# A clustered-attention kernel: masks turned earlier, conversions moved to a head's begin, and the value scale found in other places

## What is computed

```
q_assign, k_assign = argmax over 16 centroids of the normalized dot products
mask   = q_assign[:, :, :, None] == k_assign[:, :, None, :]
scores = where(mask, q k^T / 8, -1e9)
attn   = exp(scores - max(scores)); attn /= sum(attn) + 1e-9
x      = attn v                        # 16 heads, put side by side: 1536 x 512
x      = x + gate * relu(x w1[e]) w2[e]           # 1st layer, one expert e per token, if x w_skip > 0
out    = gate * sigmoid(x w_out[e]) * relu(x w1[e]) w2[e]       # 2nd layer
```

## Time and profile before

| | |
|---|---|
| median of 3 runs | 782.02 us |
| the profiled execution | 782.19 us |
| its span in the trace | 780.5 us |
| TensorE matmul busy | 713.3 us |
| VectorE busy | 447.1 us |
| ScalarE busy | 342.0 us |
| GpSimd busy | 277.7 us |
| first exponential of head 0 | 39.26 us |
| first exponential of head 15 | 347.07 us |
| last of attention on VectorE (L506) starts | 360.31 us |

### The profile page before, as it was taken

The page is one execution under the profiler, slowest core; times in us unless marked ns, Lnnn a source line. Parts: engine busy times, 40 slices in busy tenths (PEclk is TensorE's granted clock), DMA queues, the critical chain, the costliest instruction groups (busy, mean ns, idle before and its releaser), DMA issues.

```text
span 780.5 us, 17315 instructions
## 1 busy us (share of the span) xinstructions
PE 713.3 (91%) x5937; PEld 587.2 (75%) x5946; DVE 447.1 (57%) x916; ACT 342.0 (44%) x681; POOL 277.7 (36%) x341
## 2 busy tenths in 40 slices
PE   7888898888888888888899999999899999999996
PEld 4566676666767666766489999985499999999985
DVE  5767757777676777755663665444734434444321
ACT  2377667776666666665321333113212321412300
POOL 2156666555555555554121222220111312121211
PEclk8999989999999999999999999999999999999998
DMA  7101111111111111289165699729246364673100
GB/s 226 42 3 41 42 42 40 40 40 40 40 40 40 40 40 40 77 321 359 47 238 195 250 343 344 243 106 334 82 148 232 146 247 160 247 262 127 41 30 28
DMA packets 45969, 105.49 MB, mean 135 GB/s; under 512 B 5459, under 2 KB 11603, under 8 KB 45936
## 3 DMA queue, kind: packets, MB, share of 16 engines
q1 hardware_dynamic: 36352, 87.60, 31.9%
q0 software_dynamic: 4544, 12.70, 5.0%
q10 hardware_dynamic: 5040, 4.77, 1.9%
HBM read 87.64 MB, written 13.11 MB: 129 GB/s over the span
## 4 chain that ended last, share of the span: by engine, by line
PE 47%; DVE 2%; DMA 2%; issue 1%; ACT 0%; POOL 0%; POOLq 0%; ACTq 0%; DVEq 0%
PE hT_ps_layer L1132 24%; PE y_ps_layer L1145 6%; PE y_ps_layer L1149 6%; PE y_ps_layer L1152 6%; PE x_turn_layer L1119 2%; DMA x<-x_mid 1%; PE hT_ps_layer L1074 1%; PE hT_ps_layer L1061 1%; PE hT_ps_layer L1059 1%; PE x_turn_layer L1049 1%; DVE row_one_hot_layer L961 0%; DMA x_tile_layer<-x_src,token_to_read_layer 0%; DMA x_mid<-y_out_layer,y_token_layer 0%; PE count_ps_layer L1049 0%; PE rank_ps_layer L1049 0%
## 5 line engine op out<-in xcount | busy, mean ns | idle before, releaser
L349 POOL TENSOR_TENSOR probs_lo<-probs,probs_hi 128x384 f16<-128x384 f32 x160 | 143.6, 922 | 151.6 <-ACT probs_hi L305 151.6
L1132 PEld LDWEIGHTS hT_ps_layer<-xT_layer,w 128*128 128x128 f32 x1664 | 189.6, 192 | 3.4 <-DVE xT_layer L994 1.3
L1132 PE MATMUL hT_ps_layer<-xT_layer,w 128*128 128x128 f32 x1664 | 190.2, 275 | 0.5 <-issue 0.5
L883 ACT ACTIVATE hT_hi_layer<-hT_ps_layer 128x512 fp32r<-128x512 f32 x52 | 31.0, 597 | 238.8 <-PE hT_ps_layer L1132 238.8
L465 DVE TENSOR_REDUCE max_halves<-turn 128x1 f32<-128x384 f32 x192 | 99.6, 553 | 48.0 <-PE turn L565 44.4
L304 ACT ACTIVATE probs<-scores 128x384 f32<-128x384 f32 x192 | 102.8, 535 | 33.0 <-PE scores L586 32.6
L305 ACT ACTIVATE probs_hi<-scores 128x384 f16<-128x384 f32 x192 | 104.5, 545 | 0.0
L604 PE MATMUL pv<-v_hi_and_one,probs_hi 128*128 128x65 f16 x576 | 63.0, 198 | 26.2 <-ACT probs_hi L305 25.3
L1021 DVE SCALAR_TENSOR_TENSOR hT_lo_layer<-hT_ps_layer,hT_hi_layer 128x512 fp32r<-128x512 f32 x52 | 34.6, 689 | 88.5 <-ACT hT_hi_layer L883 77.4
L565 PE MATMUL turn<-kB,qB 96*128 96x384 f32 x192 | 79.1, 422 | 3.0 <-DVE max_halves L465 1.5
L878 ACT ACTIVATE w_hi<-w 128x1024 fp32r<-128x1024 f32 x64 | 62.4, 1046 | 27.0 <-issue 27.0
(11 more groups left out here) (214 smaller groups left out, 1100.5 us busy)
## 6 DMA issues: line engine op xcount, KB each, us to landing
w<-in_moe_w_dram SPq DMA_DIRECT2D x32, 2048.0 KB, 9.3
w<-in_v_dram ACTq DMA_DIRECT2D x4, 768.0 KB, 5.7
qk_raw<-in_q_dram SPq DMA_DIRECT2D x16, 192.0 KB, 2.7
qk_raw<-in_k_dram SPq DMA_DIRECT2D x16, 192.0 KB, 2.8
qB<-qA SPq DMA_DIRECT2D x16, 192.0 KB, 2.7
kB<-kA SPq DMA_DIRECT2D x16, 192.0 KB, 3.1
x_src<-x SPq DMA_DIRECT2D x2, 1536.0 KB, 11.2
x_mid<-x SPq DMA_DIRECT2D x2, 1536.0 KB, 14.4
```

The costliest lines, as they stand in the source:

```text
L349: nc.gpsimd.tensor_tensor(p_lo[slot][:, half], probs[slot][:, half], p_hi[slot][:, half], ALU.subtract).then_inc(p_lo_pool, 1)
L1132: t = nc.tensor.matmul(hp[n][:, i * P:(i + 1) * P], W1[par][:, c, f * P:(f + 1) * P], xT[:, c, :], start=(c == 0), stop=(c == CD - 1))
```

## The change

- TensorE: in each key tile the high weighing of both halves comes first, then the scores of tile kt+2, then the low weighing of tile kt-1; before, low and high weighing alternated and the scores came last. The table `BETWEEN` has other numbers: the masks are turned after scores 2 (before: after tile 1's high weighing), the first two maxima stand after scores 3 and the low weighing of tile 0 (before: behind tile 2's high weighing), maxima 2 to 5 are in tile 2, 6 to 8 in tile 3, 9 to 11 in tile 4, all four `turn_a` in tile 5, `turn_m` after it.
- ScalarE: `split_v(s+1)` and `hi(s+2)` stand at the begin of a step, ahead of its exponentials. An exponential of one column is put before the steps.
- VectorE: `split_v(s+1)` stands at the begin of a step, ahead of the copy of the turned masks.
- GpSimd: `lo_q(s+2)` first, then tile 0, `lo_k(s+2)`, tile 1, `add_up(s-1)`, tiles 2 to 4.
- SyncE: a step loads head s+3 at its begin, then doubles head s+2; its loop ends one pair of steps earlier and four steps are written out.
- Value scale: three quarters' maxima stand ahead of the first masks, the fourth and its widening right behind them; the column is turned into the PSUM tile of the cluster logits behind the first `turn_b`, and the scale's steps follow the first head's maxima. ScalarE may go on after six of the nine steps.
- More `warm` matmuls at the start: 24 instead of 20, 5 after the centroids are turned, 3 before the first `assign`.

```diff
-    BETWEEN = ((0, 0, 0, 0, 0), (0, 0, 0, 1, 0), (0, 0, 0, 1, 1), (1, 0, 1, 1, 1), (1, 1, 1, 1, 0), (1, 1, 1, 0, 0))
-    WARM_START, WARM_MASKS, WARM_TURNED, WARM_MAX = 20, 12, 6, 8
+    BETWEEN = ((0, 0, 1, 0, 0), (0, 0, 0, 0, 2), (1, 1, 1, 0, 1), (1, 0, 1, 0, 1), (1, 0, 1, 0, 1), (1, 1, 1, 1, 0))
+    WARM_START, WARM_CEN, WARM_ASSIGN, WARM_MASKS, WARM_TURNED, WARM_MAX = 24, 5, 3, 12, 6, 8
...
@@ sync
             def step(s, par):
+                if has(s, 3):
+                    load(s + 3, 1 - par)
                 if has(s, 2):
-                    if not (isinstance(s, int) and s < 0):
-                        load(s + 2, par)
                     double_hi(s + 2, par)
-            run(sp, step)
+            run(sp, step, 2)
@@ scalar
+            act.wait_ge(cen_done, 3)
+            nc.scalar.activation(v_top[:, 7:8], cen_s[:, 1:2], ACT.Exp).then_inc(exp_known, 1)
+
             def step(s, par):
                 first = isinstance(s, int) and s < 0
+                if has(s, 1) and not first:
+                    split_v(s + 1, 1 - par)
+                if has(s, 2):
+                    hi(s + 2, par)
                 for kt in range(T):
...
-                    if kt == 2 and has(s, 2):
-                        hi(s + 2, par)
-                    if kt == 3 and has(s, 1) and not first:
-                        split_v(s + 1, 1 - par)
                 if has(s, 2):
                     evac_a(s + 2, par)
+                if first:
+                    split_v(0, 0)
                 if has(s, 1):
...
-                if first:
-                    split_v(0, 0)
@@ gpsimd
                 c, a = has(s, 0), has(s, 2)
+                if a:
+                    lo_q(s + 2, par)
                 if c:
                     rest(s, 0)
+                if a:
+                    lo_k(s + 2, par)
+                if c:
                     rest(s, 1)
                 if c and not (isinstance(s, int) and s == 0):
                     add_up(s - 1)
                 if c:
-                    rest(s, 2)
-                if a:
-                    lo_q(s + 2, par)
-                if c:
-                    rest(s, 3)
-                if a:
-                    lo_k(s + 2, par)
-                if c:
-                    rest(s, 4)
+                    for kt in range(2, T - 1):
+                        rest(s, kt)
@@ vector
+            def v_widest():
                 dve.wait_ge(v_topped, QUARTERS)
                 link = link_from(dve, v_topped, QUARTERS)
                 link(nc.vector.tensor_reduce(v_top[:, 4:5], v_top[:, 0:QUARTERS], AX.X, ALU.max))
                 link(nc.vector.tensor_scalar(v_wide[:], ident[:], 0.0, v_top[:, 4:5], ALU.mult, ALU.add))
+
+            def v_power():
+
                 dve.wait_ge(v_turned, 1)
-                link(nc.vector.tensor_reduce(v_top[:, 5:6], pv[:, 0:P], AX.X, ALU.max))
+                link = link_from(dve, v_topped, QUARTERS + 2)
+                link(nc.vector.tensor_reduce(v_top[:, 5:6], lgp[:, 0:P], AX.X, ALU.max))
...
                 link(nc.vector.tensor_copy(v_bits[:, 1:2], v_scale[:, 1:2]))
+                dve.sem_inc(v_scaled, 1)
...
-                dve.sem_inc(v_scaled, 1)
...
-            v_topmost(0)
+            for n in range(3):
+                v_topmost(n)
             masks(0, 0)
-            v_topmost(1)
+            v_topmost(3)
+            v_widest()
 
             def step(s, par):
                 first = isinstance(s, int) and s < 0
                 if has(s, 1):
                     i = s + 1
+                    if not first:
+                        split_v(i, 1 - par)
...
-                        if u == 5 and first:
-                            v_topmost(2)
-                        if u == 9 and not first:
-                            split_v(i, 1 - par)
...
-                    v_topmost(3)
                     v_power()
@@ tensor
+            warm(WARM_CEN)
...
+                if isinstance(i, int) and i == 1:
+                    pe.wait_ge(v_topped, QUARTERS + 3)
...
             def turn_v():
+
                 pe.wait_ge(v_topped, QUARTERS + 2)
-                nc.tensor.transpose(pv[:, 0:P], v_wide[:], ident[:]).then_inc(v_turned, 1)
+                pe.wait_ge(mask_steps, 1)
+                nc.tensor.transpose(lgp[:, 0:P], v_wide[:], ident[:]).then_inc(v_turned, 1)
 
             for n in range(4):
                 turn_a(0, 0, n)
+            warm(WARM_ASSIGN)
...
-                between += [lambda: warm(WARM_TURNED)] if first else []
+                between += [turn_v, lambda: warm(WARM_TURNED)] if first else []
...
                 for kt in range(T):
-                    for half in range(2):
-                        if c and kt > 0:
-                            weigh_lo(s, par, kt - 1, half)
-                        other(BETWEEN[kt][2 * half])
-                        if c:
-                            weigh_hi(s, par, kt, half)
-                        if half == 0:
-                            other(BETWEEN[kt][1])
-                    other(BETWEEN[kt][3])
+                    if c:
+                        weigh_hi(s, par, kt, 0)
+                    other(BETWEEN[kt][0])
+                    if c:
+                        weigh_hi(s, par, kt, 1)
+                    other(BETWEEN[kt][1])
                     if c and kt + 2 < T:
                         scores(s, par, kt + 2, last)
+                    other(BETWEEN[kt][2])
+                    if c and kt > 0:
+                        weigh_lo(s, par, kt - 1, 0)
+                    other(BETWEEN[kt][3])
+                    if c and kt > 0:
+                        weigh_lo(s, par, kt - 1, 1)
                     other(BETWEEN[kt][4])
...
-                if first:
-                    turn_v()
```

More of the change, by code:

```diff
@@ L126, in attention @@
     cen_turned = sem("cen_turned")
+    exp_known = sem("exp_known")
     cen_ready = sem("cen_ready")
@@ L186, in wait, with run @@
             eng.wait_ge(s, value)
-    def steps(step):
+    def run(eng, step, pairs_after=1):
         step(-1, 1)
@@ L192, in steps @@
         step(1, 1)
-        def rolled(eng):
-            with eng.Fori(1, HEADS // 2 - 1) as j:
-                step(2 * j, 0)
-                step(2 * j + 1, 1)
-        yield rolled
-        step(HEADS - 2, 0)
-        step(HEADS - 1, 1)
-    def run(eng, step):
-        for rolled in steps(step):
-            rolled(eng)
+        with eng.Fori(1, HEADS // 2 - pairs_after) as j:
+            step(2 * j, 0)
+            step(2 * j + 1, 1)
+        for s in range(HEADS - 2 * pairs_after, HEADS):
+            step(s, s % 2)
     def has(s, ahead):
@@ L409, in v_topmost @@
                                         apply_absolute_value=True).then_inc(v_topped, 1)
-            def v_power():
+            def v_widest():
                 dve.wait_ge(v_topped, QUARTERS)
```

## The result

The changed kernel takes 754.69 us, median of four runs (753.46 to 757.17), against 782.53 us for the kernel before, measured beside it (four runs, 781.92 to 784.25): ratio 0.9645, 95% interval 0.9613 to 0.9676. The forecast was 746.0 us with a range of 737 to 759: 36.0 us were forecast, and the kernel got 27.8 us faster. A second measurement on another chip gave 753.23 us, ratio 0.964 (0.9605 to 0.9675).

The account below looks back on a forecast made before the run. The prediction took a chain of handovers between engines, 20.27 us a head, as the bound. Fifteen heads at 2.1 us (31.5), start 4.2 and end 0.3 gave 36.0 us off 782.0: 746.0 us, range 737 to 759.

Parts of the forecast that it names:

- E: A head's first exponential, the zero from which the prediction counts times within that head.
- first rival: TensorE: scores between the products hold up the reductions, 0.9 us more idle time a head; 759.5 us, chance 0.15.
- Part 1: TensorE's order: turned masks and first product earlier, v_lo out of the reductions; 2.12 us a head, bounds 1.4 to 2.6.
- Part 2 and 3: Conversions and v_hi at a head's begin, hidden in ScalarE's idle time; loads three heads ahead as condition; cost 0 each.
- Part 4: The start: value scale's wait and table load moved ahead or beside; gain 4.2 us, bounds 3.4 and 4.8.
- Part 5: The end, last head: scores 5 no longer wait behind tile 2's low part; gain 0.3 us, bounds 0 and 0.7.
- The conversions fit: Denies a rival: ScalarE's conversions end after E in each head, 1.1 us lost; 762.5 us, chance 0.05.
- The clock as the slower rival: TensorE's granted clock falls in every head, 53 dips cost 39.8 us; 785.8 us, chance 0.03 for slower.

Follow-up runs that it names:

- v_lo back: Changed kernel with v_lo on VectorE back at its old place behind the tenth reduction: 750.93 us, ratio 0.9628.
- old order: Changed kernel with the old order on TensorE (old table and loop), all other parts left in: 775.48 us, ratio 0.9922.
- new order alone, filler: Kernel before with only the new TensorE order, plus 16 matmuls on zeros ahead of each head's first `turn_a`: 766.48 us, ratio 0.9804.
- loads two heads ahead: Changed kernel with loads two heads ahead, as before, and conversions left at a head's begin: 796.45 us, ratio 1.0193.
- the transpose later: Changed kernel with the value scale's transpose behind the six warm matmuls instead of ahead of them: 752.03 us, ratio 0.9615.
- the order alone: Kernel before with only the changed kernel's TensorE order (table and loop), no filler: 776.62 us, ratio 0.9939.
- v_lo by GpSimd: Changed kernel with v_lo subtracted by GpSimd from a float32 copy of scaled v that ScalarE also writes: 782.16 us, ratio 0.9996.

## Why the prediction was right, and where it was too good

Heads at full clock, in us from E:

| | v_lo | copy | first reduction | last ends | next E |
|---|---|---|---|---|---|
| before | 0.61, among reductions | 3.99 | 7.27 | 14.79 | 20.27 |
| forecast | 1.06, ahead | 3.95 | 5.45 | 12.67 | 18.15 |
| changed | 1.34, ahead | 4.20 | 5.84 | 13.27 | 18.71 |
| v_lo back | 0.64, among | 3.58 | 5.22 | 13.05 | 18.51 |
| old order | 1.35, ahead | 4.17 | 7.26 | 14.42 | 19.88 |
| new order alone, filler | 1.59, among | 3.60 | 5.25 | 14.03 | 19.50 |

The measured 754.69 us lies in the stated range of 737 to 759, but above the 741 to 753 that the forecast gave as its own, between it and the first rival (759.5). The bounds of parts 1, 4 and 5 do not give 741 to 753 either: they give 737.5 to 757.6.

- **Part 1 (2.12 us a head) had the right mechanism and too large a size.** Both waits went because the masks are turned as soon as they exist and the first product follows the copy; with the old order the turned masks came at E+3.99 and the first reduction at E+7.26 again. Measured at full clock: 1.56 us, inside the bounds of 1.4 to 2.6. The 0.56 us too much are three small terms. v_lo took 1.34 us beside a busy GpSimd, above the upper bound of 1.1, so the copy came at +4.20 and not +3.95. From the copy's start to the first reduction it is 1.64 us, not the 1.50 taken: TensorE began its product 0.24 us after the copy's end, where the sum left 0.05. From the first reduction to the end of the last it is 7.43 us, not 7.22: the idle stretches came as forecast (0.31 and 0.61 for 0.35 and 0.55), but the twelve reductions fill 6.51 us of it, where I had 6.32 left over from the rows of before. The 5.48 us behind the last reduction stayed (5.44). The upper bound of 2.6 is also 0.1 below its own terms (2.12 + 0.35 + 0.23).
- The sum over fifteen heads was 31.5; 28.17 came. Of these 15 x 1.56 = 23.4 are the table's; the other 4.8 lie in heads with dips and in the first and last ones, where the kernel before lost more to the clock. The sum had no term for them. Without them the time would have been 759.5, just outside the range, so the hit is luck in part; the start, 3.3 us short of what it gave at full clock, worked the other way.
- **Part 2 and 3 (0)** were right in that nothing is late: 0.81 us of idle time is left ahead of E. "If the cover were missing it would cost up to 1.35 us a head" priced the instructions alone. With the loads two heads ahead they also waited 3.16 us for a load, and a head cost about 3 us more. And the 0 hid what the new places are good for, as the rows of the two kernels with v_lo among the reductions read: the new list of GpSimd moves GpSimd's subtractions for the coming head towards the head's begin, and without that v_lo among the now earlier reductions runs beside GpSimd. (No run moved these subtractions alone.) I priced each part with the others in place, and did not see that they cannot be added one by one.
- **Part 4 (4.2) failed in this execution, at 1.04 us.** Its cost side was "0 us, or at half clock up to 0.6 us" for three matmuls. It had no term for the value scale's transpose, at which TensorE stood 1.64 us (worth 0.4 us at full clock: 0.90 us from the copy to the first reduction with v_lo back, 0.53 with the transpose later), nor for the opening, whose 24 matmuls on zeros held the turning of the centroids to 9.20 us (with 20 of them it was 6.94), nor for a clock that falls over 20 to 26 us and slows all that leads to the first reduction. Where it did not fall there, the same start code gave first exponentials of 34.90 and 34.87, gains of 4.4 us against 39.26; where it did, 38.22, 38.12, 37.33 and 37.23, gains of 1.0 to 2.0. The 4.4 is no proof of the 4.2: the kernel before ran its own start at half clock from 10.8 to 17.6 us and from 27.9 to 31.3 us.
- **Part 5 (0.3)** was 0.0, within its bounds. The experts take 0.8 us more in the changed kernel; over the profiles of this case, none of which edits them, they take 420.2 to 422.6 us.
- **The rivals.** The scores between the products did not take the wait's place: 0.92 us of idle time in two places, near the 0.90 forecast. What lies between the forecast and this rival's time is v_lo, the start and the other terms above. The conversions fit. The clock as the slower rival, far from true for this change, is what happened to its parts: the order alone left a clock of 0.93 and lost some 6 us to it, and v_lo by GpSimd, with 0.86, lost the whole gain. Why the clock fell with those lists and not with others stays open.

The Trainium skill ("GPSIMD Engine Reference", 1. Specifications) says that GpSimd shares its SBUF interfaces with VectorE, and that instructions of VectorE with two SBUF inputs contend for them. This case's traces agree in each place: v_lo 1.34 and 1.59 us against 0.61, the comparisons 1.07 and 0.95 against 0.36. The slowdown is 0.6 to 1.0 us for an instruction, about its own length or more.

## What to carry to other kernels

Measure a stage from one head's first exponential to the next, in heads at full clock, and move what stands ahead of a handover on that chain. Here the reordering of TensorE's queue removed the waits, and the other moves kept what lay beneath them (a slow v_lo, a lower clock) from taking their place. Before moving an instruction with two SBUF inputs, look at what GpSimd does at the time where it will land, also when it only lands elsewhere because its neighbours became faster. And price parts of a change together: two parts of 5 and 6 us made 28, and much of the difference could be read from two rows, the duration of v_lo and the clock of the stretch.

## What the runs showed of the hardware

- Two-input instructions on VectorE beside a working GpSimd: 384 elements 0.61 to 1.34 and 1.59 us, 192 elements 0.36 to 1.07 us. The reductions, whose input lies in PSUM, did not slow down: four took 2.12 us at 200.28 in the new order with filler, all beside GpSimd, which works there without a break, and two took 1.01 us where it had ended.
- TensorE's clock answered to small edits elsewhere. With 16 matmuls on zeros a head it was 0.99 instead of 0.93 in the middle of the kernel, and the time 766.48 us instead of 776.62 us, though they compute nothing that is used. In another order it was 1.00 instead of 0.94, and the median was the same.
- The same instructions at the start gave a first exponential at 34.9 or at 38.2 us, with a clock of 1.00 or 0.54 from 20 to 26 us, and with 7.03 or 8.05 us for the 24 matmuls that open it. A single profile of a start is no measure of an edit of a microsecond.
